# Order of the matmuls in the output projection of a fused attention and MLP kernel: passes outside, token blocks inside

## The chip, the cores and the metric

The kernel runs on one core of a Trainium2 chip. The metric is the device time of one execution in microseconds (us), lower is better. TensorE, VectorE, ScalarE, GpSimd and SyncE appear in the profile as PE (with its weight loads as PEld), DVE, ACT, POOL and SP.

## What is computed

Attention over pooled keys and values feeds one MLP, whose result feeds a second one. All arithmetic is float32.

```python
def _attn_ref(q, k, v):                      # q, k, v: 8 batches, 8 heads, 576 tokens, 64
    k_p, v_p = (a.reshape(B, H, 72, 8, D).mean(axis=3) for a in (k, v))
    scores = 1/sqrt(D) * q @ k_p.T
    attn = softmax(scores)
    return attn @ v_p

x = attention output as (4608 tokens, 512)
h = maximum(maximum(x @ w1, x @ w2), x @ w3)   # 512 -> 768
x2 = h @ w_mid                                  # 768 -> 512
h = x2 @ w_in                                   # 512 -> 2048
g = h - tanh(h)
out = g @ w_out                                 # 2048 -> 512
```

## The kernel before

The program has two phases. The first computes attention and the first MLP batch by batch and leaves x2 in DRAM. The second, with which the change is concerned, goes over the 4608 tokens in 9 tiles of 512 (`NT`, `TB`). For each tile it computes the 2048 hidden columns in 16 chunks of 128 (`MC2`), applies g = h - tanh(h) to each chunk, and projects it.

**Three passes.** To keep float32 accuracy, each operand of a matmul is split into a high and a low part of type fp32r, and each product is made of three matmuls: high by high, high by low, low by high. `split_passes()` (L436) returns these three pairs. All three accumulate into the same place.

**`hidden(t, m)`** (L571) makes chunk m of tile t: 4 row blocks of x2 by 3 passes, 12 matmuls (L582) of 128x128 weights and 128x512 moving data, all into one accumulator bank, 4 + m % 4. It signals `h_filled`.

**`project(t, m)`** (L587) adds chunk m to the output. The 512 tokens of the tile are 4 blocks of 128 (`SUB`), j = 0 to 3, and block j accumulates in bank j over all 16 chunks. There are 4 blocks by 3 passes, 12 matmuls (L596): the 128 tokens of block j of `g` are the stationary operand, a 128x512 slice of `w_out_s` the moving one. At the first chunk of a tile (m = 0) the matmuls into bank j must wait until the previous tile's result was copied out of it (`out_drained[j]`, L594). At the last chunk (m = 15) the last matmul of each block signals `out_filled` (L600), a single semaphore that counts blocks in the order j = 0 to 3.

**Order on PE.** `tile` (L604) alternates the two by hand: project(t, m), then hidden(t, m + 3) (`LAG`), which from m = 13 on is chunk m - 13 of the next tile. So between a tile's last projection and the next tile's first one there are 12 matmuls of hidden(t+1, 2) and no others:

```python
for m in range(MC2):
    project(t, m)
    if m + LAG < MC2: hidden(t, m + LAG)
    elif ahead:       hidden(t + 1, m + LAG - MC2)
```

**Order on ACT and DVE.** Each has a hand-written `chunk(t, m)`: ACT makes squares and tanh (L783, L784, L791) and the high part of g (L777), DVE the rest (L977 to L987) and the low part of g (L966), on which the projection waits (`g_ready`). The copies of a finished tile out of the accumulator, `drain_out(t - 1)`, stand on both engines behind chunk(t, 1). ACT copies blocks 0 and 1 (L801), DVE blocks 2 and 3 (L994), each when `out_filled` has counted up to its block; each signals `out_drained[j]`. SP waits for `out_drained[j]` in the order of j and stores the block to DRAM (L378). Behind the last tile there is no further chunk: the drains wait for the last projection directly, and the program ends with the four stores.

Of the kernel before, what the change touches and what calls it, by code (L numbers as in the profile page):

```python
# [46 lines left out]
MC2 = FF2 // P  # L47
SUB = TB // P
# [70 lines left out]
def fused_attention_mlps(nc, q, k, v, w1, w2, w3, w_mid, w_in, w_out, out):  # L119
# [4 lines left out]
    with ExitStack() as ctx:  # L124
        def sem(name):
            return ctx.enter_context(nc.semaphore(name))
# [117 lines left out]
        out_filled = sem("out_filled")  # L244
        out_drained = [sem(f"out_drained{j}") for j in range(SUB)]
# [7 lines left out]
        def wait_piece(eng, i):  # L253

            if i in BY_DVE:
                eng.wait_ge(pieces_by_dve, i - BY_DVE[0] + 1)
            else:
                eng.wait_ge(pieces_by_pool, i + 1 if i < BY_DVE[0] else i + 1 - len(BY_DVE))
# [176 lines left out]
        def _(pe):  # L435
            def split_passes():  # L436

                return ((0, 0), (0, 1), (1, 0))
# [148 lines left out]
            def project(t, m):  # L587
                s = MC2 * t + m
                pe.wait_ge(g_ready, s + 1)
                if m % 4 == 0:  # L590
                    wait_piece(pe, NA + order_b.index(("out", m // 4)))
                for j in range(SUB):
                    if m == 0 and not (isinstance(t, int) and t == 0):
                        pe.wait_ge(out_drained[j], t)  # L594
                    for gs, ws in split_passes():
                        mm = pe.matmul(psum[:, j, :], g[:, m % 4, gs, j * P:(j + 1) * P],  # L596
                                       w_out_s[:, m // 4, ws, m % 4, :],
                                       start=(m == 0 and gs + ws == 0), stop=(m == MC2 - 1 and gs == 1))
                    if m == MC2 - 1:
                        mm.then_inc(out_filled, 1)  # L600

            parity = [0]

            def tile(t, odd, ahead):  # L604
                first = isinstance(t, int) and t == 0
                for m in range(MC2):
                    project(t, m)
                    if m + LAG < MC2:
                        parity[0] = odd
                        if not (first and m == 0) and not (not ahead and m + LAG == MC2 - 1):  # L610
                            hidden(t, m + LAG)
                        if not ahead and m + LAG == MC2 - 2:
                            hidden(t, MC2 - 1)
                    elif ahead:
                        parity[0] = 1 - odd
                        hidden(t + 1, m + LAG - MC2)
# [420 lines left out]
```

## Time and profile before

| | |
|---|---|
| median of 3 runs | 1603.51 us (1602.66 to 1605.18) |
| profiled execution, first to last instruction (its span) | 1601.1 us, 25315 instructions |
| PE busy | 1555.5 us (97% of the span) |
| DVE busy | 999.5 us (62%) |
| ACT busy | 600.0 us (37%) |
| granted TensorE clock over the span | 0.99 of full speed |
| second phase, about 850 us to the end | PE busy 737.6 of 740.0 us in 850 to 1590 us |
| L596 (projection), all | 1728 matmuls, 418.9 us busy |
| L582 (hidden), all | 1728 matmuls, 414.5 us busy |

The times come from one profiled execution, and no time of its own outside the span is recorded for it; the median of the plain runs lies 2.4 us above the span. In the profile's timeline a row gives the start, the duration, the engine, the line and the operation; consecutive alike instructions are one row with their count. The end of a matmul is modelled, so that the durations of successive matmuls overlap; the distance of two starts is what one matmul costs in a stream.

### The profile page before, as it was taken

What the parts mean: (1) busy time and instruction counts of PE and PEld (TensorE: products, weight loads), DVE (VectorE), ACT (ScalarE), POOL (GpSimd) and SP (SyncE); (2) the same over time, 40 slices, a digit from 0 to 9 for tenths busy, and PEclk for the clock granted to TensorE, in tenths of its full rate; (3) what the DMA queues carried; (4) which work ended last, traced back from release to release, by engine and by line L of the source; (5) the groups of instructions that cost most, each with busy time, mean ns of one, the idle gap of its engine ahead of it and who ended that gap; (6) DMA issues with size and microseconds to landing.
All of it is one profiled execution on the core that took longest, in us unless ns stands there. A gap on an engine that the chain in (4) does not pass through costs nothing.

```text
span 1601.1 us, 25315 instructions
## 1 busy us (share of the span) xinstructions
PE 1555.5 (97%) x9824; PEld 1402.6 (88%) x9824; DVE 999.5 (62%) x1604; ACT 600.0 (37%) x1119; POOL 70.9 (4%) x38
## 2 busy tenths in 40 slices
PE   3999999999999999999988999999999999999999
PEld 3899999999999999999977888888888888888887
DVE  6776464646647465433377667667667676676766
ACT  3423333223232332232354444443444444444433
POOL 2500000000000000002022000000000000000000
PEclk9999999999999999999999999999999999999999
DMA  8441122211122222001230101000000001010000
GB/s 205 116 113 40 32 56 59 59 49 42 42 49 54 54 64 68 9 20 57 79 109 1 53 1 53 0 28 26 26 26 26 27 14 39 0 53 1 27 1 27
DMA packets 70197, 72.22 MB, mean 45 GB/s; under 512 B 40016, under 2 KB 48208, under 8 KB 70128
## 3 DMA queue, kind: packets, MB, share of 16 engines
q1 hardware_dynamic: 66384, 56.63, 12.8%
q0 software_dynamic: 3744, 14.68, 2.8%
q8 instruction: 41, 0.67, 0.2%
q14 instruction: 28, 0.23, 0.0%
HBM read 52.43 MB, written 18.87 MB: 45 GB/s over the span
## 4 chain that ended last, share of the span: by engine, by line
PE 90%; DVE 6%; ACT 1%; issue 1%; DMA 1%; SPq 0%; DVEq 0%; ACTq 0%
PE psum L527 27%; PE psum L596 24%; PE psum L582 23%; PE psum L541 9%; PE psum L473 2%; PE psum L497 2%; PE psum L483 2%; DMA v_raw<-in_v 1%; PE psum L460 1%; DVE k_pooled L841 1%; DVE g L966 1%; DVE v_sum L841 0%; DVE probs L861 0%; DVE row_sum L877 0%; DVE poly L977 0%
## 5 line engine op out<-in xcount | busy, mean ns | idle before, releaser
L527 PE MATMUL psum<-x,w 128*128 128x288 f32 x3456 | 475.6, 297 | 1.6 <-DVE x L870 1.2
L527 PEld LDWEIGHTS psum<-x,w 128*128 128x128 f32 x3456 | 463.1, 189 | 5.0 <-DVE x L870 1.4
L596 PE MATMUL psum<-w_out_s,g 128*128 128x512 f32 x1728 | 418.9, 392 | 10.3 <-DVE g L966 10.3
L596 PEld LDWEIGHTS psum<-w_out_s,g 128*128 128x128 f32 x1728 | 326.6, 189 | 80.1 <-DVE g L966 11.9
L977 DVE SCALAR_TENSOR_TENSOR poly<-poly,u_sq 128x512 f32<-128x512 f32 x144 | 102.1, 709 | 236.7 <-ACT poly L791 236.7
L783 ACT ACTIVATE u_sq<-psum 128x512 f32<-128x512 f32 x144 | 86.1, 598 | 427.2 <-PE psum L582 427.2
L582 PE MATMUL psum<-x_even,w_in_s 128*128 128x512 f32 x960 | 230.0, 389 | 0.0
L582 PEld LDWEIGHTS psum<-x_even,w_in_s 128*128 128x128 f32 x960 | 180.1, 188 | 37.5
L582 PE MATMUL psum<-x_odd,w_in_s 128*128 128x512 f32 x768 | 184.5, 389 | 0.0
L582 PEld LDWEIGHTS psum<-x_odd,w_in_s 128*128 128x128 f32 x768 | 144.1, 188 | 29.9
L541 PE MATMUL psum<-h,w_mid_s 128*128 128x288 f32 x1152 | 160.8, 297 | 0.0
L541 PEld LDWEIGHTS psum<-h,w_mid_s 128*128 128x128 f32 x1152 | 154.7, 188 | 2.4
L705 ACT ACTIVATE h<-best 128x288 fp32r<-128x288 f32 x96 | 42.6, 444 | 292.5 <-DVE best L896 292.5
L891 DVE TENSOR_TENSOR best<-psum,first_copy 128x288 f32<-128x288 f32 x96 | 43.5, 453 | 106.3 <-PE psum L527 105.5
L791 ACT ACTIVATE poly<-u_sq,shift_col 128x512 f32<-128x512 f32 x144 | 104.2, 724 | 9.9 <-DVE g L966 9.9
L966 DVE TENSOR_TENSOR g<-poly,g 128x512 fp32r<-128x512 f32 x144 | 103.6, 719 | 6.3 <-ACT g L777 1.5
L987 DVE COPY_PREDICATED poly<-is_big,psum 128x512 f32<-128x512 uint8 x144 | 104.9, 728 | 0.1
L983 DVE TENSOR_TENSOR psum<-psum,tanh_h 128x512 f32<-128x512 f32 x144 | 99.6, 691 | 0.0
L981 DVE SCALAR_TENSOR_TENSOR poly<-poly,psum 128x512 f32<-128x512 f32 x144 | 98.0, 680 | 0.0
L777 ACT ACTIVATE g<-poly 128x512 fp32r<-128x512 f32 x144 | 90.9, 631 | 5.0 <-DVE poly L987 5.0
L896 DVE TENSOR_TENSOR best<-psum,best 128x288 f32<-128x288 f32 x96 | 44.0, 458 | 73.9 <-PE psum L527 72.0
L784 ACT ACTIVATE tanh_h<-psum 128x512 f32<-128x512 f32 x144 | 85.4, 593 | 0.0
(60 smaller groups left out, 1107.1 us busy)
## 6 DMA issues: line engine op xcount, KB each, us to landing
q_raw<-in_q SPq DMA_DIRECT2D x48, 192.0 KB, 2.8
x_scratch<-x_stage SPq DMA_DIRECT2D x64, 144.0 KB, 1.8
x_raw<-x_scratch SPq DMA_DIRECT2D x9, 1024.0 KB, 5.2
out<-out_stage SPq DMA_DIRECT2D x36, 256.0 KB, 2.1
v_raw<-in_v SPq DMA_DIRECT2D x15, 576.0 KB
k_raw<-in_k SPq DMA_DIRECT2D x14, 576.0 KB
stage_a<-in_moe_w POOLq DMA_DIRECT2D x6, 768.0 KB, 6.7
stage_b<-in_moe_w_out POOLq DMA_DIRECT2D x4, 1024.0 KB, 6.6
```

The lines of the kernel that those rows point to most:

```text
L527: mm = pe.matmul(psum[:, bank, 0:NH], w123[:, ws, n, c, m * P:(m + 1) * P], x[:, xs, c, h * NH:(h + 1) * NH], start=(c == 0 and ws + xs == ...
L541: mm = pe.matmul(psum[:, bank, 0:NH], w_mid_s[:, ws, m, c * P:(c + 1) * P], h1[h][:, xs, m, :], start=(m == 0 and ws + xs == 0), stop=(m = ...
L582: mm = pe.matmul(psum[:, 4 + m % 4, :], w_in_s[:, ws, c, m * P:(m + 1) * P], xs_tile[:, xs, c, :], start=(c == 0 and ws + xs == 0), stop=( ...
L596: mm = pe.matmul(psum[:, j, :], g[:, m % 4, gs, j * P:(j + 1) * P], w_out_s[:, m // 4, ws, m % 4, :], start=(m == 0 and gs + ws == 0), sto ...
L777: nc.scalar.activation(g[:, m % 4, 0, :], poly[:, m % 2], ACT.Copy).then_inc(g_hi_ready, 1)
L783: nc.scalar.activation(u_sq[:, m % 2], bank, ACT.Square).then_inc(sq_done, 1)
L791: nc.scalar.activation(poly[:, m % 2], u_sq[:, m % 2], ACT.Square, bias=shift_col[:, 0:1])\
L966: nc.vector.tensor_tensor(g[:, m % 4, 1, :], poly[:, m % 2], as_f32(g[:, m % 4, 0, :]), ALU.subtract).then_inc(g_ready, 1)
L977: nc.vector.scalar_tensor_tensor(out=p, in0=p, scalar=OFFSET, in1=u, op0=ALU.add, op1=ALU.mult)\
L981: nc.vector.scalar_tensor_tensor(out=p, in0=p, scalar=C2, in1=bank, op0=ALU.mult, op1=ALU.mult)
L983: nc.vector.tensor_tensor(bank, bank, tanh_h[:, m % 2], ALU.subtract).then_inc(dve_step, 1)
L987: nc.vector.copy_predicated(p, is_big[:, m % 2], bank).then_inc(h_drained, 1)
```

## The change

In `project` the loops over the passes and over the token blocks change places. Before, the three passes of a block followed each other into one bank, and the bank changed every third matmul. Now one pass goes over the four blocks, and each matmul writes another bank than the one ahead of it. The wait for `out_drained[j]` stands ahead of the first matmul into bank j, as before, and the signal `out_filled` is put on the last pass's matmul of each block. Number and operands of the matmuls stay.

```diff
-                for j in range(SUB):
-                    if m == 0 and not (isinstance(t, int) and t == 0):
-                        pe.wait_ge(out_drained[j], t)
-                    for gs, ws in split_passes():
+                for gs, ws in split_passes():
+                    for j in range(SUB):
+                        if gs + ws == 0 and m == 0 and not (isinstance(t, int) and t == 0):
+                            pe.wait_ge(out_drained[j], t)
                         mm = pe.matmul(psum[:, j, :], g[:, m % 4, gs, j * P:(j + 1) * P],
                                        w_out_s[:, m // 4, ws, m % 4, :],
                                        start=(m == 0 and gs + ws == 0), stop=(m == MC2 - 1 and gs == 1))
-                    if m == MC2 - 1:
-                        mm.then_inc(out_filled, 1)
+                        if m == MC2 - 1 and gs == 1:
+                            mm.then_inc(out_filled, 1)
```

On PE at the start of a tile (project(t, 0), the rows of L596; behind it hidden(t, 3), L582), with the semaphores that each instruction waits for, - is before and + is now:

```order
 L596 MATMUL psum<-w_out_s,g 128x512 [waits out_drained0,pieces_by_pool,g_ready]
-L596 MATMUL psum<-w_out_s,g 128x512 x2
 L596 MATMUL psum<-w_out_s,g 128x512 [waits out_drained1]
-L596 MATMUL psum<-w_out_s,g 128x512 x2
 L596 MATMUL psum<-w_out_s,g 128x512 [waits out_drained2]
-L596 MATMUL psum<-w_out_s,g 128x512 x2
 L596 MATMUL psum<-w_out_s,g 128x512 [waits out_drained3]
-L596 MATMUL psum<-w_out_s,g 128x512 x2
+L596 MATMUL psum<-w_out_s,g 128x512 x8
 L582 MATMUL psum<-x2_odd,w_in_s 128x512 [waits h_drained]
```

The four waits stood ahead of the 1st, 4th, 7th and 10th matmul of the group; they now stand ahead of the 1st, 2nd, 3rd and 4th. In the last chunk of a tile the four `out_filled` signals, which were on the 3rd, 6th, 9th and 12th matmul, are on the 9th, 10th, 11th and 12th. The other engines' instructions and their order are the same.

## Rows read from the trace of the kernel before

**Rows 1.** The page, busy time, share of the span and instructions by engine.
```profile
PE 1555.5 (97%) x9824; PEld 1402.6 (88%) x9824; DVE 999.5 (62%) x1604; ACT 600.0 (37%) x1119; POOL 70.9 (4%) x38
```
**Rows 2.** Groups by line, 1000 to 1540 us: xcount | busy, mean ns | idle before.
```profile
L596 PE MATMUL psum<-w_out_s,g 128*128 128x512 f32 x1189 | 285.7, 389 | 0.0
...
L582 PE MATMUL psum<-x_even,w_in_s 128*128 128x512 f32 x619 | 148.7, 389 | 0.0
```
**Rows 3.** Timeline of PE, 1126 to 1203 us: start, duration, line, count.
```profile
1126.52 2.88 PE L596 MATMUL psum<-w_out_s,g 128*128 128x512 f32 x12
1129.24 2.88 PE L582 MATMUL psum<-x_odd,w_in_s 128*128 128x512 f32 x12
1131.96 2.88 PE L596 MATMUL psum<-w_out_s,g 128*128 128x512 f32 x12
```
**Rows 4.** Timeline of PE, third and fourth matmul of one projection.
```profile
1203.13 0.39 PE L596 MATMUL psum<-w_out_s,g 128*128 128x512 f32 x1
...
1203.36 0.39 PE L596 MATMUL psum<-w_out_s,g 128*128 128x512 f32 x1
```
**Rows 5.** PE, a projection at half clock: two timeline rows, and the window with PEclk.
```profile
853.38 1.05 PE L596 MATMUL psum<-w_out_s,g 128*128 128x512 f32 x2
...
854.66 1.05 PE L596 MATMUL psum<-w_out_s,g 128*128 128x512 f32 x2
...
852.30:855.20 2.90, 2.84 (x7) 2.26 (x8) 2.69 (x6) 1.24 (x2) 0.00 (x0) 0.50 0.00 0
```
**Rows 6.** Timeline around a change of tile, 1161 to 1174 us.
```profile
1164.60 2.88 PE L596 MATMUL psum<-w_out_s,g 128*128 128x512 f32 x12
...
1166.90 1.08 ACT L801 ACTIVATE out_stage<-psum 128x512 f32<-128x512 f32 x2
...
1167.32 2.88 PE L582 MATMUL psum<-x_even,w_in_s 128*128 128x512 f32 x12
...
1169.40 0.73 DVE L987 COPY_PREDICATED poly<-is_big,psum 128x512 f32<-128x512 uint8 x1
1170.02 1.27 DVE L994 COPY out_stage<-psum 128x512 f32<-128x512 f32 x2
1170.04 2.88 PE L596 MATMUL psum<-w_out_s,g 128*128 128x512 f32 x12
1170.23 0.60 ACT L783 ACTIVATE u_sq<-psum 128x512 f32<-128x512 f32 x1 [2.25 <-PE psum L582]
```
**Rows 7.** Timeline of DVE and of PE at the last change of tile.
```profile
1518.18 1.27 DVE L994 COPY out_stage<-psum 128x512 f32<-128x512 f32 x2
...
1518.20 1.07 PE L596 MATMUL psum<-w_out_s,g 128*128 128x512 f32 x4
```
**Rows 8.** Line L994: duration min/median/max, first and last start.
```profile
L994 DVE COPY out_stage<-psum x18: 673/679/693, 908.9 to 1597.9; 128x512 f32<-128x512 f32 x18
```
**Rows 9.** Timeline of the last 11 us.
```profile
1594.09 0.69 DVE L966 TENSOR_TENSOR g<-poly,g 128x512 fp32r<-128x512 f32 x1 [0.77 <-ACT g L777]
1594.83 2.62 PEld L596 LDWEIGHTS psum<-w_out_s,g 128*128 128x128 f32 x12 [0.74 <-DVE g L966]
1594.83 3.04 PE L596 MATMUL psum<-w_out_s,g 128*128 128x512 f32 x12 [0.32 <-DVE g L966]
1595.84 1.29 ACT L801 ACTIVATE out_stage<-psum 128x512 f32<-128x512 f32 x2 [1.85 <-PE psum L596]
1596.46 2.50 SPq L378 DMA_DIRECT2D out<-out_stage  x4
1597.22 1.38 DVE L994 COPY out_stage<-psum 128x512 f32<-128x512 f32 x2 [2.44 <-PE psum L596]
```
**Rows 10.** Timeline, second matmul of the last projection.
```profile
1595.17 0.40 PE L596 MATMUL psum<-w_out_s,g 128*128 128x512 f32 x1
```
**Rows 11.** Windows at the end: us, PE, PEld, DVE, ACT, POOL busy, PEclk, DMA share, GB/s.
```profile
1597.25:1600.25 3.00, 0.62 (x3) 0.19 (x1) 1.35 (x2) 0.00 (x0) 0.00 (x0) 1.00 0.94 350
1598.00:1600.00 2.00, 0.00 (x0) 0.00 (x0) 0.60 (x1) 0.00 (x0) 0.00 (x0) 1.00 0.97 362
```
**Rows 12.** PE behind two longer stops: timeline rows, and windows with PEclk.
```profile
813.52 1.67 PE L596 MATMUL psum<-w_out_s,g 128*128 128x512 f32 x6 [0.58 <-DVE g L966]
...
828.57 4.62 PE L596 MATMUL psum<-w_out_s,g 128*128 128x512 f32 x12 [3.83 <-DVE g L966]
...
812.00:820.00 8.00, 7.42 (x33) 5.80 (x32) 5.66 (x10) 3.71 (x5) 3.30 (x1) 1.00 0.00 0
828.50:834.00 5.50, 5.43 (x17) 4.33 (x18) 4.24 (x8) 1.25 (x2) 0.53 (x1) 0.69 0.60 191
```

## The prediction

> **What bounds the kernel now.** I read the busy times first: PE is busy for 97% of the span, DVE for 62%, ACT for 37% [rows 1]. Next the groups by line in the middle of the second phase: neither the projection's matmuls (L596) nor those of the hidden chunks (L582) have any idle time ahead of them [rows 2]. So in that phase nothing but PE's own stream counts. A matmul that gets cheaper gives its whole saving, and any stop of PE is paid in full, since no slack follows in which it could be made up. The other engines matter only where PE would have to wait for them.
>
> The timeline of PE then gives the price of a matmul. A projection of 12 starts every 5.44 us, 2.72 us after it a hidden chunk of 12, 2.72 us after that the next projection [rows 3]. That is 2.72 / 12 = 0.227 us from start to start. The reader is to see that both kinds take the same 2.72 us although they use the banks differently: a hidden chunk writes one bank 12 times, while a projection changes its bank ahead of the 1st, 4th, 7th and 10th matmul. Inside one projection the third matmul (bank 0) starts at 1203.13 and the fourth (bank 1) at 1203.36 us, again 0.23 us apart [rows 4].
>
> **What the alternation of banks is worth.** If a matmul into the bank of the one before it cost more than one into another bank, a projection, with at least three changes that a hidden chunk lacks, would be shorter. The two starts agree to the last printed place, 0.01 us, which leaves at most 0.003 us for one change. Before, 8 of a projection's 12 matmuls follow one into the same bank; now none does. There are 1728 / 12 = 144 projections, so 8 x 144 = 1152 matmuls change their kind. At 0.003 us each that bounds the effect at 3.5 us either way, and I take 0, which is what all the rows read. The loads of weights change too: before, the first two passes of a block loaded the same block of g one behind the other; now each load is another one. L582 never loads the same block twice running and has the same pace, so this also costs 0.
>
> **What the waits cost at a change of tile.** Here the order of the four waits meets the DVE copies. Before a tile's first projection, bank 2 and then bank 3 are copied out by DVE: two copies from 1170.02, together 1.27 us, so bank 3 is free at 1171.29 us, and bank 2 one copy of 0.68 us [rows 8] after the start, at 1170.70. The projection starts at 1170.04 [rows 6]. Before, bank 2 was wanted by its 7th matmul, 6 x 0.227 later, at 1171.40, and bank 3 by the 10th, at 1172.08: slack of 0.70 and 0.79 us, and no idle. Now bank 2 is wanted by the 3rd matmul, at 1170.49, and bank 3 by the 4th, at 1170.72. The first is 0.21 us short; the second 1171.29 - 1170.72 = 0.57 us short, which contains the first. Banks 0 and 1 are copied by ACT from 1166.90 to 1167.98 us, 2 us ahead of their use, and stay covered.
>
> What comes on top is the restart. The last projection shows one: the DVE instruction that it waits for ends at 1594.09 + 0.69 = 1594.78, and the matmul starts at 1594.83, 0.05 later. Its group of 12 lasts 3.04 us against 2.88 us of an unbroken one [rows 6, 9], 0.16 more, of which 0.11 lies at the second matmul (it starts at 1595.17, 0.34 behind the first [rows 10], where 0.227 is usual). So one change of tile costs 0.57 + 0.05 + 0.16 = 0.78 us. The nine matmuls behind the stop and hidden(t, 3) stand in the same queue and move by as much; everything that waits for them moves along.
>
> Does DVE move its copies with the change? It makes them behind its part of chunk (t+1, 1), directly after L987 [rows 6], and that chain hangs on a hidden chunk that PE finished ahead of the old tile's last projection. So no. The last change of tile has the same picture, copies from 1518.18 and the projection from 1518.20 [rows 7]; the 18 copies of L994 are two for each of 9 tiles, hence 8 changes. **8 x 0.78 = 6.2 us.** Bounds: without the restart's 0.16, 8 x 0.62 = 5.0; with a second restart's 0.11 at bank 2, 8 x 0.89 = 7.1.
>
> One rule speaks for the lower end. At the rows' restart the weight load starts together with its matmul at 1594.83, not in the idle time ahead of it [rows 9]. The Trainium skill ("TensorE: Matmul & The Clock Gate", Back-to-back issue gap and the spec table) says that the engine pulls weight loads ahead of matmuls in flight; if the fourth load were done during the stop, the sum would be 5.0 instead of 6.2. The trace disagrees where the wait holds load and matmul alike, so I stay with 6.2.
>
> **The signals at the end of a tile.** `out_filled` now reaches 1 at the 9th matmul instead of the 3rd. Inside the program that is hidden: the 9th starts 8 x 0.227 behind 1164.60, at 1166.41, and ends by 0.39 later [rows 4] at 1166.80, while ACT comes to its copy only at 1166.90 [rows 6]. Cover 0.1 us. If it were gone, ACT would begin later, but it idles 2.25 us ahead of its next task [rows 6], so still nothing.
>
> Behind the last tile nothing hides it. ACT waits for PE 1.85 us and copies bank 0 from 1595.84; SP issues the four stores from 1596.46 on [rows 9]. From 1597.25 to 1600.25 the DMA engines move 350 GB/s at a share of 0.94 [rows 11]: 3.0 us at that rate are 1.05 MB, just the four stores of 256 KB, so the end is set by the DMA engines from the first store on. Bank 0 now is complete 6 matmuls later, 6 x 0.23 = 1.4 us. The stores then come closer together and run at the full 362 GB/s [rows 11], 2.9 us instead of 3.0: **+1.3 us**. Bounds: DVE's last copy alone moves by 0.46 us (bank 2 is complete two matmuls later than before, and DVE copies 2, then 3), so at least 0.5; at most 1.5.
>
> **Sum:** 0 + 6.2 + 1.3 = +7.5 us on a profiled span of 1601.1 us. The median of the plain runs is 2.4 us over that span, and I carry the difference over: 1603.5 + 7.5 = **1611.0 us**, 0.47% slower. A measurement of this kernel can tell some 0.2% (3.2 us) from no change. The forecast's own range is 5.0 + 0.5 to 7.1 + 1.5, give or take the run's 1 us: 1608 to 1613.
>
> **Rivals.**
>
> *The same bank does cost (ends faster).* At half clock (granted 0.50) matmuls start 0.427 us apart: three steps from 853.38 to 854.66 [rows 5]. Half of this would be 0.213, yet at full clock the step is 0.227, so 0.013 us of each matmul does not scale with the clock. If that were a pause between two writes to one bank, 1152 matmuls would lose it: -15.4 + 7.5, some 1595.6 us. Against it: then the hidden chunks would take 0.04 us longer than the projections, and rows 3 show them alike. The Trainium skill ("TensorE: Matmul & The Clock Gate", Wait — 56ns, not 53.3ns?) has only some 2.5 ns of fixed cost on top of the columns at full clock, 216 ns for 512 columns; by it 0.011 us of this kernel's step wants another explanation, and the gain would be 12.7 us instead of 15.4. Point from which it decides: a pause of 7.5 / 1152 = 0.0065 us would pay for the stops. Chance 0.05.
>
> *The stops are hidden (ends within 0.2%).* PE's early start on the next group, or copies that in fact free the bank sooner than the profile's ends say, would let the four matmuls through; only the tail's 1.3 us stays: 1604.8 us. For it: the copies' ends are measured, but the semaphore's time is not shown. Against: L966 to L596 shows the release behind the end, not ahead of it [rows 9]. DVE would have to be 0.6 us earlier. Chance 0.14.
>
> *The change does nothing (order without effect, signals where they were).* The order of instructions shows the waits at the 1st to 4th matmul, so this has 0.01, at 1603.5 us.
>
> *The clock falls (slower still).* Behind a stop of 3.83 us the granted clock was down to 0.69 of full speed over 5.5 us, and 12 matmuls took 4.62 us; behind one of 0.58 us it stayed at 1.00 [rows 12]. The new stops are like the second. If each cost what the first did behind its stop, 4.62 - 2.88 = 1.7 us, the sum would be 8 x 1.7 = 14 us more, 1625 us. Chance 0.02.
>
> **Chances.** Forecast 0.78, hidden stops 0.14, bank gain 0.05, no effect 0.01, clock 0.02. The range starts at 1604.3 us, to hold the case of hidden stops, and ends at 1614.0 us, to hold the upper bounds and part of the 3.5 us left for the banks. Faster by over 0.2%: 0.05. Within 0.2%: 0.15 (hidden stops and no effect). Slower by over 0.2%: 0.80.
>
> **What would show it.** Timeline at a change of tile: three matmuls of L596, or two, then a gap of about 0.5 us put down to DVE L994, then nine or ten; eight such gaps, some 4 to 5 us of idle ahead of L596 in its group row. Starts within a projection still 0.227 us apart, 2.72 for 12. The four stores at the end issued from about 1.4 us after the position they had relative to the last projection, and closer together. I am wrong if a projection in the middle of a tile takes less than 2.70 us, or if no idle time stands ahead of L596 at the changes of tile.

## The result and the profile after

The changed kernel takes 1611.75 us in the median of three runs (1611.04 to 1611.89), the kernel before 1603.51 us: 1.0048 times as long, 95% interval 1.0032 to 1.0064. The forecast was 1611.0 us. The profiled execution has a span of 1609.2 us, 8.1 more than that of before.

The page of the changed kernel, the rows of the projection and of the hidden chunks. Columns: count, busy us, mean ns of one, idle us of the engine ahead of them and what ended most of it.

```profile
L596 PE MATMUL psum<-w_out_s,g 128*128 128x512 f32 x1728 | 424.4, 394 | 11.9 <-DVE g L966 10.3
L596 PEld LDWEIGHTS psum<-w_out_s,g 128*128 128x128 f32 x1728 | 326.7, 190 | 86.9 <-DVE g L966 12.0
L582 PE MATMUL psum<-x_even,w_in_s 128*128 128x512 f32 x960 | 230.2, 389 | 0.0
```

Same number of matmuls and loads; 5.5 us more busy time in L596 (418.9 before), 1.6 us more idle, and nothing to speak of for L582 (230.0 before in this group). The idle column says little here: the end of a matmul is modelled 0.39 us behind its start while the starts are 0.227 us apart, and a matmul behind a wait is drawn longer. A stop of 0.6 us therefore shows mostly as busy time. The distance of starts is the thing to read.

The timeline of the changed kernel at the change of tile that answers to rows 6:

```profile
1167.68 2.88 PE L596 MATMUL psum<-w_out_s,g 128*128 128x512 f32 x12
...
1169.99 1.08 ACT L801 ACTIVATE out_stage<-psum 128x512 f32<-128x512 f32 x2
...
1170.40 2.88 PE L582 MATMUL psum<-x_even,w_in_s 128*128 128x512 f32 x12
1172.49 0.73 DVE L987 COPY_PREDICATED poly<-is_big,psum 128x512 f32<-128x512 uint8 x1
...
1173.11 1.27 DVE L994 COPY out_stage<-psum 128x512 f32<-128x512 f32 x2
1173.12 3.63 PE L596 MATMUL psum<-w_out_s,g 128*128 128x512 f32 x12
...
1173.84 0.19 PEld L596 LDWEIGHTS psum<-w_out_s,g 128*128 128x128 f32 x1 [0.53 <-DVE out_stage L994]
1174.44 1.90 PEld L596 LDWEIGHTS psum<-w_out_s,g 128*128 128x128 f32 x9 [0.41 <-DVE out_stage L994]
```

The first projection of the tile now lasts 3.63 us instead of 2.88. Its third load starts at 1173.84, 0.05 behind the end of DVE's first copy (1173.11 + 0.68), its fourth at 1174.44, 0.06 behind the end of the second (1173.11 + 1.27); the matmuls of both loads start with them. ACT's and DVE's copies stand where they stood from the start of the old tile's last projection: 2.31 and 5.43 us behind it, 2.30 and 5.42 before [rows 6].

The rows that answer to rows 3, in the middle of a tile:

```profile
1179.32 2.88 PE L596 MATMUL psum<-w_out_s,g 128*128 128x512 f32 x12
1182.04 2.88 PE L582 MATMUL psum<-x_even,w_in_s 128*128 128x512 f32 x12
1184.76 2.88 PE L596 MATMUL psum<-w_out_s,g 128*128 128x512 f32 x12
```

A projection is 2.72 us from its start to the next group's, as before, though now each of its matmuls changes the bank. Last, the end of the program (rows 9), and the DMA engines there in the windows view (us, PE, PEld, DVE, ACT, POOL busy, PEclk, DMA share, GB/s):

```profile
1601.72 3.02 PE L596 MATMUL psum<-w_out_s,g 128*128 128x512 f32 x12 [0.32 <-DVE g L966]
1604.10 1.08 ACT L801 ACTIVATE out_stage<-psum 128x512 f32<-128x512 f32 x2 [3.23 <-PE psum L596]
1604.55 1.29 DVE L994 COPY out_stage<-psum 128x512 f32<-128x512 f32 x2 [2.88 <-PE psum L596]
1604.72 1.81 SPq L378 DMA_DIRECT2D out<-out_stage  x4
```
```profile
1605.50:1608.40 2.90, 0.00 (x0) 0.00 (x0) 0.34 (x1) 0.00 (x0) 0.00 (x0) 1.00 0.97 362
```

ACT waits 3.23 us for the first complete bank instead of 1.85, and SP issues the four stores from 3.00 us behind the start of the last projection instead of 1.63, within 1.8 us instead of 2.5. From the start of the last projection to the end of the span it is 1609.2 - 1601.7 = 7.5 us; before it was 1601.1 - 1594.8 = 6.3.

So the 8.1 us of the two spans divide as follows. From DVE's first copy of a finished tile (908.9 before, 909.7 now) to the start of the last projection: 685.9 us before, 692.0 now, +6.1, in which the eight changes of tile lie. The end: +1.2. The rest, +0.8, was there before the first copy: two projections behind the long waits near 828 and 852 us take 5.49 and 5.22 us instead of 4.62 and 5.02, and the phase began 0.3 us earlier. At the first of them PE's clock fell sooner: in 829 to 830 us the granted share is 0.50 here and was 0.69 before. This does not follow the order of the matmuls. Of the runs below, two have the old order at this projection: with the first chunk alone it takes 5.44 us, with the last chunk alone 4.45. The changed kernel with ACT's copies has the new order there and takes 4.61. The first copy of a finished tile starts at 910.3, 908.6 and 910.7 us in the first three runs below. I take the 0.8 us for chance.

### The profile page after: what moved, and what is told of

Read it like the earlier page. It is cut to its first block, busy times and chain, and to the rows that moved or that the text cites. A ratio compares the mean times of both kernels' runs of the same rounds, so it can differ in the third digit from the quotient of the medians.

```text
span 1609.2 us, 25315 instructions
## 1 busy us (share of the span) xinstructions
PE 1561.2 (97%) x9824; PEld 1403.2 (87%) x9824; DVE 999.1 (62%) x1604; ACT 600.1 (37%) x1119; POOL 71.0 (4%) x38
## 4 chain that ended last, share of the span: by engine, by line
PE 88%; DVE 6%; issue 2%; ACT 1%; DMA 1%; SPq 0%; DVEq 0%; ACTq 0%
PE psum L527 28%; PE psum L596 22%; PE psum L582 22%; PE psum L541 9%; PE psum L473 2%; PE psum L497 2%; PE psum L483 2%; DMA v_raw<-in_v 1%; PE psum L460 1%; DVE poly L981 1%; DVE out_stage L994 1%; DVE psum L983 1%; DVE g L966 1%; ACT poly L791 1%; DVE poly L977 1%
## 5 line engine op out<-in xcount | busy, mean ns | idle before, releaser
L596 PE MATMUL psum<-w_out_s,g 128*128 128x512 f32 x1728 | 424.4, 394 | 11.9 <-DVE g L966 10.3
L596 PEld LDWEIGHTS psum<-w_out_s,g 128*128 128x128 f32 x1728 | 326.7, 190 | 86.9 <-DVE g L966 12.0
L977 DVE SCALAR_TENSOR_TENSOR poly<-poly,u_sq 128x512 f32<-128x512 f32 x144 | 102.2, 710 | 243.6 <-ACT poly L791 243.6
L582 PE MATMUL psum<-x_even,w_in_s 128*128 128x512 f32 x960 | 230.2, 389 | 0.0
L582 PEld LDWEIGHTS psum<-x_even,w_in_s 128*128 128x128 f32 x960 | 180.4, 188 | 37.5
L582 PE MATMUL psum<-x_odd,w_in_s 128*128 128x512 f32 x768 | 184.5, 389 | 0.0
L582 PEld LDWEIGHTS psum<-x_odd,w_in_s 128*128 128x128 f32 x768 | 144.2, 188 | 29.9
L966 DVE TENSOR_TENSOR g<-poly,g 128x512 fp32r<-128x512 f32 x144 | 103.7, 720 | 6.3 <-ACT g L777 1.5
L983 DVE TENSOR_TENSOR psum<-psum,tanh_h 128x512 f32<-128x512 f32 x144 | 99.8, 693 | 0.0
```

The source lines that it names most:

```text
L582: mm = pe.matmul(psum[:, 4 + m % 4, :], w_in_s[:, ws, c, m * P:(m + 1) * P], xs_tile[:, xs, c, :], start=(c == 0 and ws + xs == 0), stop=( ...
L966: nc.vector.tensor_tensor(g[:, m % 4, 1, :], poly[:, m % 2], as_f32(g[:, m % 4, 0, :]), ALU.subtract).then_inc(g_ready, 1)
L977: nc.vector.scalar_tensor_tensor(out=p, in0=p, scalar=OFFSET, in1=u, op0=ALU.add, op1=ALU.mult)\
L983: nc.vector.tensor_tensor(bank, bank, tanh_h[:, m % 2], ALU.subtract).then_inc(dve_step, 1)
```

## The experiments

Theory: the alternation of banks is worth nothing; the loss is eight stops on DVE's copies (6.1 us) and a longer end (1.2 us). Rivals: the order of the matmuls costs something by itself; the four waits cost something by standing close together. Each run is compared with runs of the kernel before on the same chip. Where the projection's loops are written as one loop over a list of (block, pass), the line numbers behind them move by 2 to 8. The code shown is the telling part of each edit; the text says where it stands against another run's code.

### The middle chunks alone

Against the changed kernel, with the loop's body left out:

```diff
-                for gs, ws in split_passes():
-                    for j in range(SUB):
+                order = [(j, gs, ws) for j in range(SUB) for gs, ws in split_passes()]
+                if 0 < m < MC2 - 1:
+                    order = [(j, gs, ws) for gs, ws in split_passes() for j in range(SUB)]
+                for j, gs, ws in order:
```

> Passes outside only in the chunks 1 to 14 of a tile; the first and the last chunk keep the order of before. This is the alternation of banks alone, on 14/16 of the projections, without any wait moved and without any out_filled signal moved. My theory (the alternation is worth nothing, all of the loss is stops and tail): 1603.5 us, ratio 1.000, and a projection in the middle of a tile takes 2.72 us from its start to the next group's start. Rival (a matmul that changes the bank is dearer or cheaper, and that makes the loss): with the whole 8.2 us in the 1152 changed steps, 7/8 of it would be here, 1610.7 us, ratio 1.0045; a hidden gain under the stops would show as a ratio under 1.

Measured: 1603.76 us against 1603.94, ratio 0.9998 (0.9989 to 1.0007). The timeline of PE in the middle of a tile:

```profile
1176.82 2.88 PE L598 MATMUL psum<-w_out_s,g 128*128 128x512 f32 x12
1179.54 2.88 PE L582 MATMUL psum<-x_even,w_in_s 128*128 128x512 f32 x12
1182.26 2.88 PE L598 MATMUL psum<-w_out_s,g 128*128 128x512 f32 x12
```

2.72 us again. The rival's 1.0045 is outside the interval. Alternation costs nothing and gains nothing that these runs can tell.

### The first chunk alone

Against the run above:

```diff
-                if 0 < m < MC2 - 1:
+                if m == 0:
```

> Passes outside only in the first chunk of a tile. This moves the four waits for out_drained to the 1st to 4th matmul and nothing else. My theory: the eight stops are here in full, 8 x 0.77 = 6.1 us, and the tail is that of before: 1609.6 us, ratio 1.0038; the distance between the DVE copies of successive tiles is 87.80 us instead of 87.04. Rival (loss from the order itself): 1/16 of it, 1604.0 us.

Measured: 1608.98 us, ratio 1.0039 (1.0025 to 1.0052). The timeline at a change of tile has the long group and an ordinary one behind it:

```profile
1172.05 3.62 PE L598 MATMUL psum<-w_out_s,g 128*128 128x512 f32 x12
1175.51 2.88 PE L582 MATMUL psum<-x_even,w_in_s 128*128 128x512 f32 x12
```

From start to start that is 3.46 us where 2.72 was, 0.74 more, and the copies of the first two finished tiles lie 87.84 us apart (908.58 and 996.42) instead of 87.04. One chunk in sixteen carries most of the loss; a rival that spreads it over the chunks expected 1604.0, which is a ratio of 1.0003 and outside the interval.

### The last chunk alone

Against the run of the middle chunks:

```diff
-                if 0 < m < MC2 - 1:
+                if m == MC2 - 1:
```

> Passes outside only in the last chunk of a tile. This moves the out_filled signals and nothing else. My theory: only the tail grows, by 1.2 us: 1604.7 us, ratio 1.0007, within what a measurement can tell, so the profile must show it: from the start of the last projection to the end of the span 7.5 us instead of 6.3, and no stop at a change of tile (distance of the copies 87.04 us). Rival (the late signals also delay ACT, and through it the next tile): more than 2 us.

Measured: 1605.42 us, ratio 1.0009 (1.0000 to 1.0018). That is too little to tell from no change by the times; the profile shows the end. Its last projection starts at 1596.62 us and its span is 1604.1, 7.5 us later, as in the changed kernel:

```profile
1596.62 3.01 PE L598 MATMUL psum<-w_out_s,g 128*128 128x512 f32 x12 [0.33 <-DVE g L968]
1598.99 1.09 ACT L803 ACTIVATE out_stage<-psum 128x512 f32<-128x512 f32 x2 [3.22 <-PE psum L598]
```

The rival, that the late signals delay ACT and through it the next tile, is not excluded by the times, whose interval reaches 1.0018 (2.9 us). The profile excludes it: the copies of the first two tiles start at 910.68 and 997.72 us, 87.04 apart as before.

The ratios of the three parts, -0.02%, +0.39% and +0.09%, add up to +0.46%; the whole change has +0.48%.

### The same four waits, with the banks free in time

This is the changed kernel with another split of the copies; shown is ACT's `drain_out`, and DVE's begins where it ends.

```diff
-                for j in range(SUB // 2):
+                for j in range(SUB // 2 if isinstance(t, int) and t == NT - 1 else SUB):
```

> The changed kernel, but at the change of tile ACT copies all four blocks out and DVE none; only after the last tile they share the copies as before. ACT is then done by 1166.9 + 4 x 0.6, about 1169.3 us, ahead of the projection at 1170.04, so that no wait is open. My theory: the stops go, the tail stays: 1603.5 + 1.2 = 1604.7 us, ratio 1.0007. Rival (the stops are not made by the copies of DVE but by the waits themselves standing close together): about 1611 us, ratio 1.0045, since all four waits still stand at the 1st to 4th matmul.

Measured: 1605.47 us, ratio 1.0009 (1.0000 to 1.0018). The timeline:

```profile
1515.53 2.06 ACT L801 ACTIVATE out_stage<-psum 128x512 f32<-128x512 f32 x4
1515.94 2.88 PE L582 MATMUL psum<-x_even,w_in_s 128*128 128x512 f32 x12
1518.66 2.88 PE L596 MATMUL psum<-w_out_s,g 128*128 128x512 f32 x12
1518.86 0.60 ACT L783 ACTIVATE u_sq<-psum 128x512 f32<-128x512 f32 x1 [1.27 <-PE psum L582]
```

ACT has copied all four blocks 1.1 us ahead of the projection and still idles 1.27 us behind it. The group is 2.72 us long from start to start. The waits stand at the 1st to 4th matmul and cost nothing, and the rival's 1.0045 is outside the interval; it was the banks that were late, not the waits that were close.

### The suspected cost doubled

Again the changed kernel; ACT copies block 0, DVE blocks 1 to 3. Shown is ACT's `drain_out`.

```diff
-                for j in range(SUB // 2):
+                for j in range(SUB // 2 if isinstance(t, int) and t == NT - 1 else 1):
```

> The changed kernel, but at the change of tile DVE copies three blocks (1, 2, 3) and ACT one; after the last tile they share as before. This doubles the suspected cost: DVE's copies start at the projection's own start and end 0.6 us apart, so bank 3 is free some 1.87 us behind it, and is wanted by the 4th matmul 0.68 us behind it. Stop: 1.19 + 0.05 + 0.16 = 1.4 us, 8 times 11.2, and 1.2 for the tail: 1615.9 us, ratio 1.0077, distance of the copies of successive tiles about 88.4 us. Rival (the stops are a fixed price of four waits close together, not set by the end of the last copy): 1611 us, unchanged.

Measured: 1616.46 us, ratio 1.0074 (1.0058 to 1.0089). The timeline:

```profile
1174.72 1.88 DVE L994 COPY out_stage<-psum 128x512 f32<-128x512 f32 x3
1174.74 0.39 PE L596 MATMUL psum<-w_out_s,g 128*128 128x512 f32 x1
...
1175.45 3.53 PE L596 MATMUL psum<-w_out_s,g 128*128 128x512 f32 x11 [0.33 <-DVE out_stage L994]
...
1178.82 2.88 PE L582 MATMUL psum<-x_even,w_in_s 128*128 128x512 f32 x12
```

The group takes 4.08 us from start to start, 1.36 more than usual, where 1.4 was expected. The third copy's 0.6 us per tile came through whole.

### Alternating banks without the stops

Against the changed kernel's order written as such a list, in every chunk:

```diff
-                    order = [(j, gs, ws) for gs, ws in split_passes() for j in range(SUB)]
+                    order = [(j, gs, ws) for pair in (0, 2) for gs, ws in split_passes()
+                             for j in (pair, pair + 1)]
```

> Every projection goes over the passes for the blocks 0 and 1 and then for the blocks 2 and 3. Each matmul still writes another bank than the one ahead of it, all three passes stay outside of a loop over blocks, but bank 2 is wanted by the 7th matmul as before and bank 3 by the 8th, at 1170.04 + 7 x 0.227 = 1171.62 us, 0.3 behind the end of its copy. My theory: no stop; in the tail bank 0 is complete with the 5th matmul instead of the 3rd, +0.46 us: 1604.0 us, ratio 1.0003. Rival (alternating banks cost or gain something by themselves): as the changed kernel, or under 1603.

Measured: 1604.21 us, ratio 0.9997 (0.9988 to 1.0007). A change of tile is undisturbed:

```profile
1519.33 1.28 DVE L996 COPY out_stage<-psum 128x512 f32<-128x512 f32 x2
1519.35 2.88 PE L598 MATMUL psum<-w_out_s,g 128*128 128x512 f32 x12
1522.07 2.88 PE L582 MATMUL psum<-x_even,w_in_s 128*128 128x512 f32 x12
```

The end, from 1595.99 us to the span's 1602.7, is 6.7 us: 0.4 more than before, 0.46 expected. A second order in which every matmul changes its bank, and again no gain; the bank is simply wanted 1.6 us into the projection instead of 0.7.

### A version that beats both

Passes outside has one property that the projection did not use: its first eight matmuls read only the high part of g. This version waits for the low part just ahead of the ninth, lets ACT make the copies, and keeps the last chunk of the last tile in the old order. The list starts out in the old order; ACT's copies are edited as in the run "The same four waits" and not shown again.

```diff
-                pe.wait_ge(g_ready, s + 1)
+                pe.wait_ge(g_hi_ready, s + 1)
...
+                if not (isinstance(t, int) and t == NT - 1 and m == MC2 - 1):
+                    order = [(j, gs, ws) for gs, ws in split_passes() for j in range(SUB)]
+                for at, (j, gs, ws) in enumerate(order):
+                    if gs == 1 and all(o[1] == 0 for o in order[:at]):
+                        pe.wait_ge(g_ready, s + 1)
```

> A version that may beat both: passes outside, so that the first eight matmuls of a projection need only the high part of g; PE waits for the high part at first and for the low part only ahead of the first matmul of the third pass. ACT copies all blocks at a change of tile (as in the run before), and the last chunk of the last tile keeps the blocks outside, which keeps the tail short. In the middle of the phase PE waits for neither, so nothing changes there. PE waits for the low part of g four times in the kernel before (10.3 us in all); the low part comes 0.7 to 0.8 us behind the high part, so up to 4 x 0.7 us go: 1600.7 to 1603.5 us, I say 1601.5, ratio 0.9988. If those waits only move to another place (the chain through ACT and DVE stays the same length): 1603.5 us, no change.

Measured: 1598.74 us against 1604.68, ratio 0.9967 (0.9955 to 0.9978), nearly three times the 2.0 us that I gave it, and about twice my upper bound of 2.8. PE's timeline at the two waits that are left:

```profile
824.00 1.98 PE L600 MATMUL psum<-w_out_s,g 128*128 128x512 f32 x8
828.52 1.21 PE L600 MATMUL psum<-w_out_s,g 128*128 128x512 f32 x4 [2.54 <-DVE g L970]
...
843.20 1.98 PE L600 MATMUL psum<-w_out_s,g 128*128 128x512 f32 x8
848.93 2.08 PE L600 MATMUL psum<-w_out_s,g 128*128 128x512 f32 x4 [3.75 <-DVE g L970]
```

Four waits, 10.3 us in all, have become two of 6.3. I had valued each wait at 0.7 us, the time between the high and the low part in the undisturbed chain. But at the two long waits the low part was several microseconds behind the high one: at the second, in the kernel before, ACT has made the high part at 843.64 us and DVE the low part at 852.30. So all eight matmuls, 1.8 us, went into the waiting time. PE's clock also fell less: over 800 to 870 us the granted share is 0.98 instead of 0.93.

### Its control, without the early start

Against the run above:

```diff
-                pe.wait_ge(g_hi_ready, s + 1)
+                pe.wait_ge(g_ready, s + 1)
...
-                for at, (j, gs, ws) in enumerate(order):
-                    if gs == 1 and all(o[1] == 0 for o in order[:at]):
-                        pe.wait_ge(g_ready, s + 1)
+                for j, gs, ws in order:
```

> The same as e7_high_first but with the wait for the low part at the head of the projection, as in the kernel before. Passes outside, ACT copies all blocks, the tail as before except for what the last chunk of the last tile finds. My theory: neither stops nor a longer tail, and the alternation of banks in nearly all projections is worth nothing: 1603.5 us, ratio 1.000. What e7_high_first is faster than this is the early start alone.

Measured: 1603.93 us, ratio 0.9998 (0.9989 to 1.0007). With the copies on ACT and the old order in the very last chunk, the change is worth nothing in either direction. The gain of the run before is the early start alone.

### The early start in the old order

Against the run with the early start:

```diff
-                    order = [(j, gs, ws) for gs, ws in split_passes() for j in range(SUB)]
+                    order = [(j, gs, ws) for j in range(SUB) for gs, ws in split_passes()]
```

The copies are again shared by ACT and DVE.

> The kernel before (blocks outside, passes inside, DVE and ACT copies as before), with only the early start of e7_high_first: PE waits for the high part of g at the head of a projection and for the low part ahead of the first matmul that reads it, which in this order is the 3rd instead of the 9th. My theory of e7's gain: at each place where PE waits for the low part, the matmuls that need only the high part are made in the waiting time, and behind the shorter wait PE's clock falls less. Then two matmuls per place instead of eight: 0.45 us at each of four places (0.32 at the last), 1.7 us in all: 1601.8 us, ratio 0.9989. Rival (the early start is worth the same in either order, since what counts is the chain through g): as e7, 1598.5 us, ratio 0.9967.

Measured: 1601.56 us against 1603.98, ratio 0.9984 (0.9975 to 0.9993). PE's timeline:

```profile
825.98 0.61 PE L598 MATMUL psum<-w_out_s,g 128*128 128x512 f32 x2
830.04 4.63 PE L598 MATMUL psum<-w_out_s,g 128*128 128x512 f32 x10 [3.44 <-DVE g L968]
```

Two matmuls ahead of the wait instead of eight, and a wait of 3.4 us instead of 2.5. This profile is of the slowest of the eleven executions (1604.25 us). The order gains 0.16% where the passes outside gain 0.33%, and the rival's 0.9967 is outside its interval; the ends of the two intervals just overlap (0.9975 and 0.9978). How the 2.4 us divide between waits and clock is not settled by one profile.

### Shorter GpSimd instructions

Against the run with the early start and the passes outside:

```diff
-                    nc.gpsimd.tensor_tensor(lo, st, as_f32(hi), ALU.subtract).then_inc(pieces_by_pool, 1)
+                    parts = st.shape[1] if i >= NA else 1
+                    for n in range(parts):
+                        rows = slice(n, n + 1) if parts > 1 else slice(None)
+                        last = nc.gpsimd.tensor_tensor(lo[:, rows], st[:, rows], as_f32(hi[:, rows]), ALU.subtract)
+                    last.then_inc(pieces_by_pool, 1)
```

> e7_high_first, and in the second phase each subtraction of GpSimd that makes the low part of a piece of weights (L426, 128x2048, 4.5 to 5.1 us) is cut into four of 128x512. In the trace of the kernel before, DVE instructions that begin beside such a subtraction last until some 0.3 to 0.6 us behind its end (4.64 instead of 0.69 us, 4.74 instead of 0.42), and the two long waits of PE hang on them. My theory of these waits: DVE is shut out for as long as one GpSimd instruction runs, so with quarters of 1.2 us it waits for 1.2 us at most each time; the two waits of 6.3 us in all shrink by half or more: some 3 us faster than e7, 1595.5 us, ratio 0.9948. Rival (the two engines share the way in to memory evenly, and only the total of bytes counts, or DVE is shut out again by the next quarter): the waits stay, 1598.5 us, ratio 0.9967.

Measured: 1597.04 us against 1604.51, ratio 0.9955 (0.9942 to 0.9969). That is the fastest median, but its interval overlaps that of the version above. The timeline is divided too:

```profile
819.16 2.99 POOL L429 TENSOR_TENSOR w_in_s<-stage_b,w_in_s 128x512 fp32r<-128x512 f32 x2
819.64 1.36 DVE L985 SCALAR_TENSOR_TENSOR poly<-poly,u_sq 128x512 f32<-128x512 f32 x1 [2.20 <-ACT poly L799]
...
823.24 4.96 POOL L429 TENSOR_TENSOR w_out_s<-stage_b,w_out_s 128x512 fp32r<-128x512 f32 x4
823.67 5.08 DVE L974 TENSOR_TENSOR g<-poly,g 128x512 fp32r<-128x512 f32 x1
...
828.81 2.07 PE L604 MATMUL psum<-w_out_s,g 128*128 128x512 f32 x4 [3.68 <-DVE g L974]
...
844.17 6.13 POOL L429 TENSOR_TENSOR w_out_s<-stage_b,w_out_s 128x512 fp32r<-128x512 f32 x4
...
845.73 1.71 DVE L974 TENSOR_TENSOR g<-poly,g 128x512 fp32r<-128x512 f32 x1
...
847.50 1.19 PE L604 MATMUL psum<-w_out_s,g 128*128 128x512 f32 x4 [0.68 <-DVE g L974]
```

In the first of these places a DVE instruction got in behind one quarter: L985 ends at 821.00 us, 0.55 behind the third quarter's end (820.45), and the fourth quarter takes 1.74 us instead of 1.29. The subtraction L974 got in the same way at 845.73: it ends 0.54 behind the second quarter (845.61 + 1.29), and the third takes 1.74. But the same L974 stayed shut out over all four quarters from 823.24 us on.

PE waits 4.4 us in two places instead of 6.3. One wait shrank from 3.75 to 0.7 us. The other grew from 2.5 to 3.7: PE comes to it 0.84 us earlier than in the run with undivided subtractions (its eight matmuls start at 823.16 instead of 824.00), and DVE's release comes 0.28 later (828.75 instead of 828.47). Theory and rival each hold at one of the places; why DVE gets in at one and not at the other is open.

## Why the prediction was right

- **Price of a matmul and of the alternation: 0.** Right. Two orders with a change of bank at every matmul have ratios of 0.9998 and 0.9997, and the projection still takes 2.72 us. The comparison inside the trace of before, three changes of bank against none at equal length [rows 3, 4], had told it.
- **Eight stops: 6.2 us.** The profiles show 6.1; the first chunk alone has a ratio of 1.0039, 6.3 us. The step that carried it was to set the end of each copy against the time at which the new order wants the bank [rows 6]. The fourth matmul was to start at 1171.34 against 1170.04 for the first, 1.30 later; it starts 1174.44 - 1173.12 = 1.32 later. From its start to the next group's the projection takes 1176.60 - 1173.12 = 3.48 us, 0.76 more than the usual 2.72, where 0.78 was forecast. Bank 2 stopped PE as well, and its restart cost nothing extra, since the next wait swallowed it: the term without a second restart was the right one.
- **The restart: 0.05 + 0.16 us.** Right, and the weight load did not run ahead: loads three and four start behind the release, not in the idle time. The sum with the load done during the stop, 5.0 us, is below the 6.1 of the profile.
- **The end: 1.3 us.** The profiles show 1.2, here and with the last chunk alone. The DMA engines move 362 GB/s over the 2.9 us from the first packets on, as assumed.
- **ACT's cover of 0.1 us** held: L801 starts 2.31 us behind the start of the old tile's last projection, 2.30 before, without a wait.
- **The rivals.** Bank gain: the 0.013 us that do not scale with the clock [rows 5] are not a pause between writes to one bank. The 11 ns by which the Trainium skill's figure ("TensorE: Matmul & The Clock Gate", Wait — 56ns, not 53.3ns?) is below this kernel's step stay unexplained, but alternating banks does not bring them back. Hidden stops: wrong. Fall of the clock: it is granted in full (1.00) from 1172 to 1177 us, around a stop.
- **One detail was wrong:** I looked for 4 to 5 us of new idle time in the projection's group row. It is 1.6, because of the modelled ends, and at the change of tile the profile prints the idle time ahead of the weight loads (0.53 and 0.41 us) and none ahead of the matmuls. The gap that I named as the sign shows at the loads alone. The distance of starts is the measure.

The two terms, 7.5 us together, stand against 7.3 in the profiles, and that is the mechanism. That the medians met as closely, +7.5 forecast and +8.2 measured, is in part luck: three executions a side leave 5.1 to 10.3 us (1.0032 to 1.0064), and the two spans hold 0.8 us that no term had.

## What to carry to other kernels

An order that touches all accumulators early and completes them all late shortens the time in which they can be copied out, at both ends. Before changing a loop order on a saturated engine, list for each buffer the time of its first use and of its last, and set them against the end of the copy and the start of the next reader. The same order pays where the operand's parts arrive at different times: put first the passes whose operand is ready, and wait for the other part only where it is read.

## What was not expected of the hardware

Some DVE instructions that run beside a GpSimd subtraction in SBUF are not slowed by a share but held until it ends. In the kernel before (timeline):

```profile
823.45 4.51 POOL L426 TENSOR_TENSOR w_out_s<-stage_b,w_out_s 128x2048 fp32r<-128x2048 f32 x1 [0.51 <-ACT w_out_s L647]
...
823.87 4.64 DVE L966 TENSOR_TENSOR g<-poly,g 128x512 fp32r<-128x512 f32 x1
...
845.53 4.56 POOL L426 TENSOR_TENSOR w_out_s<-stage_b,w_out_s 128x2048 fp32r<-128x2048 f32 x1 [0.36 <-ACT w_out_s L647]
845.63 4.74 DVE L979 TENSOR_SCALAR is_big<-u_sq 128x512 uint8<-128x512 f32 x1
```

L966 takes 0.69 us elsewhere and ends here 0.55 us behind GpSimd's end; L979 takes 0.42 us elsewhere and ends 0.28 us behind it. These two are what PE's waits of 3.8 and 5.5 us in the start of the phase hang on. It is not every DVE instruction: L983, which reads one operand from PSUM and one from SBUF, runs from 823.15 us across the start of the first subtraction in its usual 0.69, and in the last run the like instructions L989 and L991 take their usual 0.67 and 0.68 us beside the quarter of 844.17 to 845.64. The held ones, L966, L979 and, with 2.55 instead of 0.69 us at 843.16, L977, read SBUF alone. It works the other way round too: a quarter that begins while DVE's L974 runs (838.27 behind 838.16 us, in the last run) takes 1.73 us instead of 1.29. The Trainium skill ("SBUF — State Buffer", Who interferes with whom) says that the two engines share a pair of ports which one instruction holds until it ends; the rows agree. Where GpSimd's instructions follow each other closely, the last run has both: one DVE subtraction waited for four of them, 5.08 us, and the same line got in behind one of them at 845.73 us.
